# Queries and keys in one buffer with one scaling operation per level, and a block-diagonal copy of each level's queries made by ScalarE

## The reference

```python
# attention: q, k, v, alpha of shape (4, 8, 768, 48)
for t in range(S):
    state = alpha[:, :, t, :, None] * state + einsum('bhd,bhe->bhde', k[:, :, t], v[:, :, t])
    y[:, :, t] = einsum('bhd,bhde->bhe', q[:, :, t], state)
x = y as (3072, 384)
# first dense part, d_ff 1536
x = (sigmoid(x @ w_gate) * (x @ w_val)) @ w_out
# second dense part: 4 experts of width 1024, weighted by normalised domain_probs
out = sum_e p[:, e:e+1] * (relu(x @ w1[e]) @ w2[e])
```

## Time and profile before

| | |
|---|---|
| median of 3 runs | 1534.03 us (1532.52 to 1534.43) |
| profiled execution, its own time | 1535.03 us |
| its span | 1533.2 us |
| granted TensorE clock, mean | 0.994 |
| PE busy | 1452.3 us, 95% |
| DVE, POOL, ACT busy | 769.7, 609.6, 382.5 us |

### The profile page before, as it was taken

The page is one execution under the profiler, slowest core; times in us unless marked ns, Lnnn a source line. Parts: engine busy times, 40 slices in busy tenths (PEclk is TensorE's granted clock), DMA queues, the critical chain, the costliest instruction groups (busy, mean ns, idle before and its releaser), DMA issues.

```text
span 1533.2 us, 25937 instructions
## 1 busy us (share of the span) xinstructions
PE 1452.3 (95%) x10296; PEld 1324.9 (86%) x10296; DVE 769.7 (50%) x1256; ACT 382.5 (25%) x687; POOL 609.6 (40%) x590
## 2 busy tenths in 40 slices
PE   2688999999999999899999999999999999999999
PEld 2577988898888989899899999999999999999998
DVE  9888586858778685921333333333333333333333
ACT  1432222323222232232222222222222222222221
POOL 6566443544545354534432422413333243142120
PEclk9989999999999999999999999999999999999999
DMA  6321221222212121111001001001010010000011
GB/s 235 124 74 66 69 77 49 80 67 80 67 51 91 46 89 49 50 42 29 14 1 37 5 0 42 0 1 41 0 41 0 0 41 0 14 27 0 0 62 62
DMA packets 41102, 69.95 MB, mean 46 GB/s; under 512 B 5936, under 2 KB 24112, under 8 KB 41008
## 3 DMA queue, kind: packets, MB, share of 16 engines
q1 hardware_dynamic: 41008, 68.64, 13.3%
HBM read 63.91 MB, written 4.72 MB: 45 GB/s over the span
## 4 chain that ended last, share of the span: by engine, by line
PE 68%; issue 14%; DVE 9%; POOL 7%; SPq 0%; DMA 0%; ACT 0%; POOLq 0%; DVEq 0%; ACTq 0%
PE PS L619 26%; PE PS L609 26%; PE PS L565 9%; DVE Q L803 4%; PE PS L575 4%; DVE K L803 2%; PE PS L512 1%; POOL TOT L990 1%; POOL row L1006 1%; POOL hs0l L1032 1%; POOL hs1l L1032 1%; DVE AT L856 1%; POOL row L999 1%; POOL row L996 1%; POOL y_near L1012 1%
## 5 line engine op out<-in xcount | busy, mean ns | idle before, releaser
L951 DVE SCALAR_TENSOR_TENSOR acc<-PS,prob,acc 128x384 f32<-128x384 f32 x192 | 118.7, 618 | 160.4 <-PE PS L619 160.4
L1063 POOL TENSOR_TENSOR XS_0l<-x2T,XS_0h 128x1536 fp32r<-128x1536 f32 x24 | 84.3, 3514 | 260.7 <-ACT XS_0h L739 260.7
L803 DVE TENSOR_TENSOR Q<-Q,TOT 48x256 f32<-48x256 f32 x280 | 184.6, 659 | 2.9 <-PE PS L516 0.9
L1063 POOL TENSOR_TENSOR XS_1l<-x2T,XS_1h 128x1536 fp32r<-128x1536 f32 x23 | 80.7, 3510 | 250.8 <-ACT XS_1h L739 250.8
L959 DVE SCALAR_TENSOR_TENSOR H_1l<-PS,H_1h 128x512 fp32r<-128x512 f32 x96 | 66.4, 692 | 195.2 <-ACT H_1h L774 195.2
L959 DVE SCALAR_TENSOR_TENSOR H_0l<-PS,H_0h 128x512 fp32r<-128x512 f32 x96 | 66.1, 691 | 187.3 <-ACT H_0h L774 187.3
L512 PEld LDWEIGHTS PS<-Q,K 112*64 112x64 f32 x1920 | 72.4, 148 | 87.5 <-issue 29.8
L512 PE MATMUL PS<-Q,K 112*64 112x64 f32 x1920 | 89.1, 239 | 59.1 <-DVE Q L803 24.9
L774 ACT ACTIVATE H_1h<-PS 128x512 fp32r<-128x512 f32 x96 | 57.4, 598 | 309.3 <-PE PS L609 309.3
L774 ACT ACTIVATE H_0h<-PS 128x512 fp32r<-128x512 f32 x96 | 57.2, 598 | 297.3 <-PE PS L609 297.1
L893 DVE TENSOR_TENSOR hid<-PS,hid 128x384 f32<-128x384 f32 x96 | 53.4, 557 | 107.6 <-PE PS L565 106.0
(11 more groups left out here) (154 smaller groups left out, 4150.4 us busy)
## 6 DMA issues: line engine op xcount, KB each, us to landing
row<-in_rows SPq DMA_DIRECT2D x24, 768.0 KB, 4.4
V<-in_v SPq DMA_DIRECT2D x24, 384.0 KB, 4.8
rawA<-in_w SPq DMA_DIRECT2D x8, 768.0 KB, 4.5
rawB<-in_w SPq DMA_DIRECT2D x8, 768.0 KB, 6.2
K<-in_k SPq DMA_DIRECT2D x24, 224.0 KB, 2.8
A<-in_alpha SPq DMA_DIRECT2D x24, 224.0 KB, 3.1
Q<-in_q SPq DMA_DIRECT2D x48, 96.0 KB, 2.9
out_y<-acc SPq DMA_DIRECT2D x5, 768.0 KB, 3.6
```

The source lines that it names most:

```text
L803: done = dve.tensor_tensor(x, x, y, ALU.mult)
L951: dve.scalar_tensor_tensor(out=acc[:, n, :], in0=PS[:, result_banks[u], 0:DM], scalar=weight, in1=acc[:, n, :], op0=ALU.mult, op1=ALU.add) ...
L1063: nc.gpsimd.tensor_tensor(XS[c % 2][1][:], x2T[:, :, at:at + T2], XS[c % 2][0][:].bitcast(F32), ALU.subtract).then_inc(xsl_ready, 1)
```

## The change

Keys and queries of a step come in one buffer `KQ[p]` of shape (partitions, 2, pairs, positions), in one DMA; the decays in a second. DVE scales both with one `tensor_tensor` per level. `Qc` goes, since half 0 of `KQ[p]` is the same thing. The block-diagonal form that the level matmuls need is now a buffer `QX[p]` of half the size of `Q[p]`, which holds only the right columns of the current level. ACT fills it before each level by two copies, one for each head (`spread_heads`), after `kq_ready` or `prep_ready`; PE waits for the new `qx_ready`. The memsets of `Q[p]` become memsets of `QX[p]`, and the loads don't wait for them. The ACT copies of the first three weight pieces move from behind level 2 of step 2's place in ACT's order to separate places among the first levels.

```diff
-            Q.append(sb(f"Q{p}", [P, PAIRS, 2, C]))
-            K.append(sb(f"K{p}", [P, PAIRS, C]))
+            KQ.append(sb(f"KQ{p}", [P, 2, PAIRS, C]))
+            QX.append(sb(f"QX{p}", [P, PAIRS, 2, HC]))
...
-                for to, x in ((K[p], at[1]), (A[p], at[2])):
-                    sp.dma_start(to[0:R], x.rearrange("r (a t) -> r a t", t=C)).then_inc(step_in[p], 16)
-                if is_first(i, sc):
-                    sp.wait_ge(q_clear, sc + 1)
-                for w, lo in ((0, 0), (1, HB)):
-                    sp.dma_start(Q[p][lo:lo + D, :, w, :], at[0][w].rearrange("d (a t) -> d a t", t=C)).then_inc(step_in[p], 16)
+                sp.dma_start(A[p][0:R], at[0].rearrange("r (a t) -> r a t", t=C)).then_inc(step_in[p], 16)
+                sp.dma_start(KQ[p][0:R], at[1].rearrange("r (s a t) -> r s a t", s=2, t=C)).then_inc(step_in[p], 16)
...
-                    if level == 0:
-                        pe.wait_ge(prep_ready, per_step(i, sc, 1, 1))
-                    else:
-                        pe.wait_ge(kq_ready, per_level(i, sc, level - 1))
+
+                    pe.wait_ge(qx_ready, per_level(i, sc, level))
...
-                        pe.wait_ge(qc_ready, per_state(i, sc, 0))
+                        pe.wait_ge(kq_ready, per_level(i, sc, LEVELS - 1))
...
+            def spread_heads(i, sc, level):
+
+
+                if level == 0:
+                    act.wait_ge(prep_ready, per_step(i, sc, 1, 1))
+                else:
+                    act.wait_ge(kq_ready, per_level(i, sc, level - 1))
+                p = buffer_of(i, sc)
+                for g, rows in enumerate((slice(0, D), slice(HB, HB + D))):
+                    right = level_columns(KQ[p][rows, 0], level)
+                    done = nc.scalar.activation(QX[p][rows, :, g, :].rearrange("d a (n t) -> d a n t", t=2 << level), right, ACT.Copy)
+                done.then_inc(qx_ready, 1)
+
+            def next_columns(i, base, kind, j, level):
+
+
+                if kind == LVL and level < LEVELS - 1:
+                    spread_heads(i, base + j, level + 1)
+                elif kind == LVL and base and not last_step(i, base + j):
+                    spread_heads(i, base + j + 1, 0)
...
                         task(i, STEPS_T * (tc + 1), *t)
+                    for t in slots[n] if n < len(slots) else []:
+                        next_columns(i, STEPS_T * (tc + 1), *t)
                     group(i, tc + nxt, kind, f)
...
+            for j in range(STEPS_T):
+                spread_heads(0, j, 0)
             for n, t in enumerate(FIRST):
                 task(0, 0, *t)
-                for m in {(LVL, 2, MASKED - 1): range(3), (LVL, 2, LEVELS - 1): (3,), (TRK, 0, 0): (4,), (TRK, 1, 0): (5,)}.get(t, ()):
+                next_columns(0, 0, *t)
+                for m in {(LVL, 1, 1): (0,), (LVL, 0, 2): (1,), (LVL, 2, 2): (2,), (LVL, 2, LEVELS - 1): (3,), (TRK, 0, 0): (4,), (TRK, 1, 0): (5,)}.get(t, ()):
                     high_raw1(m)
...
-                ops = []
-                if k_too:
-                    left = halves(K[p][0:R], h)[:, :, :, 0, :]
-                    ops.append((left, spread(tot[0:R, :, :, 1], h)))
-                if q_too:
-                    for w, rows in heads:
-                        right = halves(Q[p][rows, :, w, :], h)[:, :, :, 1, :]
-                        ops.append((right, spread(tot[rows, :, :, 0], h)))
-                for x, y in ops:
-                    done = dve.tensor_tensor(x, x, y, ALU.mult)
-                done.then_inc(kq_ready, 1)
+                both = KQ[p][0:R].rearrange("r s a t -> r (s a t)")
+                tot = TOT[p][h][0:R].rearrange("r a m -> r (a m)").rearrange("r (k s) -> r s k", s=2)
+                if k_too and q_too:
+                    x, y = both[:, h:2 * PAIRS * C - h].rearrange("r (s m t) -> r s m t", s=2, t=h)[:, :, 0::2, :], tot
...
+                y = y.unsqueeze(len(y.shape)).to_broadcast(list(x.shape))
+                dve.tensor_tensor(x, x, y, ALU.mult).then_inc(kq_ready, 1)
...
-                nc.vector.memset(Q[p][:], 0.0).then_inc(q_clear, 1)
+                nc.vector.memset(QX[p][:], 0.0)
...
-                if (kind, level) == ((LVL, LEVELS - 1) if base else (TRK, 0)):
-                    if sc % CHUNKS:
-                        wait_count(pool, y_done, per_step(i, sc, 1, 0 if sc % CHUNKS > 1 else -1))
-                        pool.wait_ge(kq_ready, per_level(i, sc, LEVELS - 1))
-                        nc.gpsimd.tensor_tensor(Qc[0:R], Q[p][0:R, :, 0, :], Q[p][0:R, :, 1, :], ALU.add).then_inc(qc_ready, 1)
-                    if base and not last_step(i, sc):
-                        decays(i, sc + 1)
+                if base and (kind, level) == (LVL, LEVELS - 1) and not last_step(i, sc):
+                    decays(i, sc + 1)
```

More of the change, by code:

```diff
@@ L199, in wait_apart, with attention_moe_program @@
         eng.sem_inc(passed, 1)
-def attention_moe_program(nc, q, k, alpha, v, rows, w_gate, w_val, w_out, probs, w1, w2, masks, eye, out):
+def attention_moe_program(nc, qk, alpha, v, rows, w_gate, w_val, w_out, probs, w1, w2, masks, eye, out):
     with ExitStack() as ctx:
@@ L499, in task @@
                 if kind == LVL:
-                    if level == 0:
-                        pe.wait_ge(prep_ready, per_step(i, sc, 1, 1))
-                    else:
-                        pe.wait_ge(kq_ready, per_level(i, sc, level - 1))
+                    pe.wait_ge(qx_ready, per_level(i, sc, level))
                     for a in range(PAIRS):
-                        cols = level_columns(Q[p][0:R, a], level)
-                        r = cols.shape[-1]
+                        cols = QX[p][0:R, a]
+                        dst = bank[:, a * C:(a + 1) * C].rearrange("s (g t) -> s g t", g=2)
                         if level < TILED:
-                            per_half = cols.shape[-2] // 2
                             for c in range(2):
-                                mine, blocks = slice(HC * c, HC * (c + 1)), slice(per_half * c, per_half * (c + 1))
-                                dst = bank[mine, a * C:(a + 1) * C].rearrange("s (g n t) -> s g n t", g=2, t=r)[:, :, blocks]
-                                mm = pe.matmul(dst, K[p][0:R, a, mine], cols[:, :, blocks], start=True, stop=True)
+                                mine, right = slice(HC * c, HC * (c + 1)), slice(HC // 2 * c, HC // 2 * (c + 1))
+                                mm = pe.matmul(dst[mine, :, right], KQ[p][0:R, 1, a, mine], cols[:, :, right], start=True, stop=True)
                         else:
                             mine = slice(HC * (a % 2), HC * (a % 2 + 1))
-                            dst = bank[mine, a * C:(a + 1) * C].rearrange("s (g n t) -> s g n t", g=2, t=2 << level)
-                            mm = pe.matmul(dst, K[p][0:R, a, 0:HC], cols, start=True, stop=True)
+                            mm = pe.matmul(dst[mine], KQ[p][0:R, 1, a, 0:HC], cols, start=True, stop=True)
                     mm.then_inc(level_done, 1)
@@ L531, in task @@
                         for mine in sides if chunk else ():
-                            pe.matmul(bank[mine, a * 2 * D:(a + 1) * 2 * D], Qc[0:R, a, mine], ST[0:R, a, :],
+                            pe.matmul(bank[mine, a * 2 * D:(a + 1) * 2 * D], KQ[p][0:R, 0, a, mine], ST[0:R, a, :],
                                       start=True, stop=False, skip_group_check=True)
@@ L811, in prepare @@
                     dve.wait_ge(step_in[p], inputs_in(i, sc))
-                    a = halves(A[p][0:R], 1)
-                    even, odd = a[:, :, :, 0, 0], a[:, :, :, 1, 0]
-                    dve.tensor_tensor(TOT[p][2][0:R], even, odd, ALU.mult).then_inc(tot2_ready, 1)
-                    left = halves(K[p][0:R], 1)[:, :, :, 0, 0]
-                    dve.tensor_tensor(left, left, odd, ALU.mult)
-                    for w, rows in heads:
-                        x = halves(Q[p][rows, :, w, :], 1)[:, :, :, 0, 0]
-                        dve.tensor_tensor(x, x, halves(A[p][rows], 1)[:, :, :, 0, 0], ALU.mult)
+                    a = A[p][0:R].rearrange("r a t -> r (a t)").rearrange("r (k s) -> r s k", s=2)
+                    dve.tensor_tensor(TOT[p][2][0:R].rearrange("r a m -> r (a m)"), a[:, 0], a[:, 1], ALU.mult).then_inc(tot2_ready, 1)
+                    even = KQ[p][0:R].rearrange("r s a t -> r s (a t)")[:, :, 0::2]
+                    dve.tensor_tensor(even, even, a, ALU.mult)
                 else:
                     dve.wait_ge(tot2_ready, per_step(i, sc, 1, 1))
-                    for w, rows in heads:
-                        x = halves(Q[p][rows, :, w, :], 1)[:, :, :, 1, 0]
-                        done = dve.tensor_tensor(x, x, TOT[p][2][rows], ALU.mult)
-                    done.then_inc(prep_ready, 1)
+                    odd = KQ[p][0:R, 0].rearrange("r a t -> r (a t)")[:, 1::2]
+                    dve.tensor_tensor(odd, odd, TOT[p][2][0:R].rearrange("r a m -> r (a m)"), ALU.mult).then_inc(prep_ready, 1)
```

31 lines of the change are left out of this document (14 added, 17 removed).

## The result

The change makes the kernel faster: 1499.17 us (median of 4 runs, 1495.96 to 1501.65) against 1533.28 us for the kernel before on the same chip (1532.07 to 1534.43), a ratio of 0.9776 with an interval of 0.9755 to 0.9797.

A forecast was written before the change was run, and what follows sets the result against it. PE fixes 57% of the span (from 660 us); before that DVE sets the start, PE the steady tiles, apart from latency between levels. Start -12, first tile -3, steady tiles -3: -18 us, from 1535.03 to 1516, range 1503 to 1534.

The forecast's parts named there:

- third rival: DVE's queue gone in the steady tiles: -12 there, -6 first tile, -14 start, 1502 us; chance 0.16.
- The merged product and the copy: Each level: one DVE product of 0.69 us, 0.91 with one wait; each ACT copy 0.42, a pair 0.83.
- The prediction's other figure, 0.51: ACT copy price by the skill's ScalarE rule: 0.51 us, a pair 1.02, making the steady-tile sum 8 us higher.
- The steady tiles: Six tiles: idle 3.2 us each against 3.5 to 4.6, so -3 us, bounds -12 and +12.
- bare gap: Between two levels, one dense group, no ACT rectangles: three per tile, 0.01 plus POOL's full 0.22 each, 0.7 together.
- The gaps with rectangles: Levels 3-4, ACT's rectangle copies ahead of the spread: two per tile, PE waits 0.36 us each.
- those behind a value group: Levels 4-5, ACT copies the value product before the rectangles: two per tile, PE waits 0.46 us each.
- The term of 0.9: Steady tiles: 0.9 us added per tile for gaps with DVE behind YOUT's work or POOL's near terms.
- The first tile: First tile with attention, 11.5 us idle: a quarter taken back, -3 us, bounds -7 and +2.
- The start: Up to the first dense matmul: -12 us, bounds -19 and -5; level 0 at about 10 us.
- `Qc` "at nothing": Steady tiles: removing `Qc` gains nothing, its 1.3 us on POOL lying while PE has dense groups.
- The rival that the new hop decides: Single-group gaps: POOL's waits don't shrink, ACT's 0.93 follows; +19 in six tiles, +3 first, 1544 us; chance 0.12.

The follow-up runs named there:

- without near terms: POOL's near-term products replaced by memsets and small operations, result incomplete: kernel before 1498.55 us (0.9755), changed kernel 1496.00 us (0.9748).
- spread first: Changed kernel with ACT's copies for the next level ahead of the rectangle copies, in the steady tiles' order: 1495.70 us, ratio 0.9746 to the kernel before.
- start too: Changed kernel with ACT's copies for the next level ahead of the rectangle copies in the start as well as the tiles: 1496.33 us, ratio 0.9745.
- weights later: Kernel of spread first, with ACT's three weight copies of the first tile moved behind three groups apart: 1495.08 us, ratio 0.9743 to the kernel before.
- Three products: Changed kernel with DVE scaling a level by three operations again, on the packed buffer, ACT's copies kept: 1575.75 us, ratio 1.0258 to the kernel before.
- copies twice: Changed kernel with ACT making each block-diagonal copy a second time into a spare buffer, in between: 1545.56 us, ratio 1.0070 to the kernel before.
- `Qc` back: Changed kernel with POOL making `Qc` again for the queries that meet the state, PE waiting for it: 1509.75 us, ratio 0.9840 to the kernel before.

## Why the prediction was wrong

The direction was right, and so was the main mechanism, that one operation is held once where three can be held three times. The size was wrong, as the waits were priced at the wrong gaps: of the cases that the prediction named, its third rival happened (DVE's relief frees the steady tiles as well: -12, -6, -14, 1502 us).

**The merged product and the copy** were sized right: 694 ns in the median against 0.69, with its waits 816 on the mean against 0.91; the copy 419 ns against 0.42. The prediction's other figure, 0.51 by the Trainium skill (ScalarE: Activation LUTs, "Rules for kernel authors"), was misapplied: the page gives it for a bias that is read from a `[128,1]` operand, and these copies name none. So the 0.42 measured here doesn't speak against that row, and the 8 us had no ground. ACT's load of 15 us per tile came out as 15.0.

**The steady tiles are the step that failed.** The text gave each bare gap "the full 0.22 of POOL", and "to this I add 0.9 for the gaps in which DVE is behind YOUT's work or POOL's near terms". After has waits of neither kind: the bare gaps show none above 0.14, and every wait of the six tiles is 0.7 or less. The gaps with rectangles came about as worked out, 0.28 to 0.56 (forecast 0.36); those behind a value group 0.45 to 0.72 in one step and at most 0.13 in the other (forecast 0.46 each). The tiles were left with 1.6 of idle time each, 1.3 of it in these waits, instead of 3.2.

The mistake was to spread a mean over all gaps. Counted from the traces, 89 products of the six steady tiles were held by over 0.1 us in the kernel before, 63 us in all, and 17 products after, 6 us. Of this, one of the three bare gaps of a tile had 0.2 us a tile, the other two nothing, and none of the three lost time by it; the earlier trace rows had shown their products at 0.42 and 0.85. Most of PE's waits fell on two places of a tile. Behind level 3 of the second step, products were held in turn (0.58, 1.04 and 1.12 in the tile of the lines below), and PE waited 0.80 to 1.57. Behind level 2 of the third step nothing was held, but DVE came to its products 2.8 to 3.0 us after the level task, as those of the level before had been held; PE waited 1.24 to 1.50:

```profile
294.27 2.18 DVE L803 TENSOR_TENSOR Q<-Q,TOT 48x256 f32<-48x256 f32 x2
296.50 0.69 PE L512 MATMUL PS<-Q,K 112*64 112x64 f32 x16 [1.45 <-DVE Q L803]
...
314.56 0.41 DVE L803 TENSOR_TENSOR K<-K,TOT 112x256 f32<-112x256 f32 x1
315.79 0.69 PE L512 MATMUL PS<-Q,K 112*64 112x64 f32 x16 [1.25 <-DVE Q L803]
```

These two places make 15.0 of the 21.8 us. After, the first waits 0.39 to 0.56, behind ACT's rectangles, and the second not at all: DVE starts 0.73 after the level task of 282.06.

```profile
282.79 0.69 DVE L812 TENSOR_TENSOR KQ<-KQ,TOT 112x512 f32<-112x512 f32 x1
```

The term of 0.9, for "the gaps in which DVE is behind YOUT's work or POOL's near terms", kept part of just these waits, and they went. The runs show it from both sides: without near terms the kernel before falls by 36 us and after by 3. One operation is held once and then has slack; three were held in turn, and the level task was late. The rule that the prediction cited on the shared pair (the Trainium skill, SBUF — State Buffer, "Who interferes with whom") is borne out by both; the 3.30 us product at 222.98 shows more than it says (last section).

**The first tile** has the same cause. "I take back a quarter, -3" was a guess without a row; it was -10.6. Near terms alone were 8.8 us there in the kernel before, and of the 10.6, 3.6 are PE's busy time, at a clock that no longer fell.

**The start** was right: -12 against -15.1 in the profiled execution. That execution started early, though: the three kernels that differ least from it up to the first dense matmul (spread first, start too, weights later) reach it at 66.1 to 66.7 us, and 65 was forecast. Of its terms, neither `prepare` (1.8 us of start when undone) nor the loads can be told from that scatter. Level 0 began at 11.3 and not at 10, and levels 3 to 5 were a little longer than before, so more came from levels 0 to 2: they took 18.1 us instead of 29.7, where the terms of the forecast made 22.5 of it. POOL's waits there had been given 2 us, too little.

**`Qc` "at nothing"** was wrong: 7 us at least, most in the first tile, though in the steady tiles, which the text named, it was 1.2. The cover of PE's dense groups held for `Qc` itself; what wasn't priced is POOL's work behind it, near products and weight splits, which the longest product of that run stands behind.

**The rival that the new hop decides** didn't happen, for its condition wasn't met: it let POOL's waits stay, and they went from 63 us to 6. Three products show what the same hop costs behind 1.19 us instead of 0.69: 77 us. With the merge the chain takes 2.3 where 2.4 are to be had. That the margin is this thin is shown by copies twice: one more pair of copies, +46 us. A product of 0.92, the forecast's upper bound, would have made PE wait in each bare gap, by my estimate from these rows 0.1 to 0.2 us.

## What to carry to other kernels

Never spread a mean wait over all the places where it could fall: list the places, look at the durations there, and give the long ones to their own gaps. Where two engines share a port, count an operation by how often it can be held and not only by its length; with three products a level POOL's near terms cost 32 to 36 us here, with one 3. A hand-over to another engine is priced against the slack of the gap that it falls into, so test a move and the change that makes room for it together: either alone would have been thrown away here.

## What the runs showed of the hardware

A DVE product was not let in between POOL operations that follow each other closely: the one of 0.42 us at 222.98 above ended at 226.28, after the fourth of POOL's operations had ended at 226.00. In `Qc` back a product begun at 118.28 ended at 124.02, behind six operations, the last until 123.47. It isn't always so: in after the product begun at 115.39 was through at 116.89, behind one operation (115.34 to 116.34), and POOL's next one, begun at 116.31, took 1.46 us where its like take 1.0. No run tells what decides it. I had reckoned with one operation of POOL as the longest wait.

TensorE's clock fell in the first tile, and less often after the change. The windows of before, and then of after:

```profile
80.00:85.00 5.00, 5.00 (x33) 4.68 (x33) 4.94 (x6) 0.98 (x2) 4.57 (x8) 0.68 0.73 142
105.00:110.00 5.00, 3.64 (x27) 3.41 (x28) 3.78 (x8) 1.07 (x2) 3.25 (x8) 0.71 0.00 0
130.00:135.00 5.00, 4.93 (x24) 4.79 (x25) 3.49 (x9) 1.25 (x3) 1.28 (x2) 0.66 0.26 102
```
```profile
60.00:65.00 5.00, 2.37 (x7) 2.40 (x8) 4.92 (x8) 0.40 (x1) 2.95 (x3) 0.54 1.01 323
65.00:70.00 5.00, 5.00 (x36) 4.68 (x35) 3.00 (x4) 2.79 (x5) 4.61 (x8) 0.78 0.74 147
70.00:75.00 5.00, 4.17 (x47) 3.46 (x47) 3.72 (x6) 2.71 (x7) 1.27 (x2) 1.00 0.00 2
```

Before, three stretches hold time at the lower level (1.2 GHz), in which matmuls of 384 columns start 0.32 us apart instead of 0.17, and two of them lie behind waits of 1.9 to 2.2 us of PE; after, only the first dense matmuls do, behind the wait of 4.0 us. After has one wait of 2.1 us in that tile too (82.34), and the clock stayed at 1.00 behind it. No run was made on this; it is read from two profiles. In three products it fell in the steady tiles too, where PE waited for 49.8 us in all.

The start differs by 3 to 4 us between executions with the same operations, along with the arrival of a step's data: in spread first DVE could begin on step 2's data at 11.30 instead of 9.97, and a product met POOL's run of near products at its beginning (3.32 us at 14.59; after had 0.72 at 13.16 and 2.44 at 14.90). A difference of that size in one profiled start is not a result.
